# Two weight loads moved ahead of a wait and a row load on SyncE's queue

## The reference

```python
# 1. attention, q k v (2, 8, 768, 64): bits of q @ proj and k @ proj give a bucket; only equal buckets attend
scores = scale * q @ k.T;  scores = where(q_bucket == k_bucket, scores, -1e9)
x = (softmax(scores) @ v).transpose(0, 2, 1, 3).reshape(1536, 512)
# 2. SwiGLU with RMS norm, d_ff = 1536
xn = x / sqrt(mean(x * x) + 1e-6) * rms_g
x = (silu(xn @ w_gate) * (xn @ w_val)) @ w_out
# 3. one expert of eight for each token, w1[e] (512, 1024), w2[e] (1024, 512)
e_idx = argmax(x @ gate);  gate_w = the chosen probability;  eom = sigmoid(x @ output_gate)
out[e_idx == e] = gate_w * eom[:, e] * (relu(x[e_idx == e] @ w1[e]) @ w2[e])
```

## Time and profile before

| | |
|---|---|
| median of 3 runs | 762.18 us (761.68 to 762.22) |
| profiled execution, its time | 762.22 us |
| its span | 760.5 us |
| TensorE matmul busy | 744.0 us, 98% |
| chain that ended last, TensorE's share | 85% |

### The profile page before, as it was taken

The page is one execution under the profiler, slowest core; times in us unless marked ns, Lnnn a source line. Parts: engine busy times, 40 slices in busy tenths (PEclk is TensorE's granted clock), DMA queues, the critical chain, the costliest instruction groups (busy, mean ns, idle before and its releaser), DMA issues.

```text
span 760.5 us, 13422 instructions
## 1 busy us (share of the span) xinstructions
PE 744.0 (98%) x4556; PEld 678.6 (89%) x4556; DVE 475.6 (63%) x930; ACT 377.0 (50%) x675; POOL 300.9 (40%) x346
## 2 busy tenths in 40 slices
PE   6999999999999999999999999999999999999996
PEld 5899899989888999999999998888899988889985
DVE  8899999999987764344434453336366654665430
ACT  5988898888898411111111123443435454455531
POOL 7778777778888654433333200111110111010111
PEclk9999999999999999999999999999999999999998
DMA  7797788688410131121111022003046767776400
GB/s 216 208 277 210 212 238 211 191 196 223 118 34 29 35 118 42 56 66 45 41 41 41 0 97 83 29 28 139 33 160 207 227 199 239 258 219 200 157 25 23
DMA packets 54677, 98.33 MB, mean 129 GB/s; under 512 B 7042, under 2 KB 21390, under 8 KB 54625
## 3 DMA queue, kind: packets, MB, share of 16 engines
q1 hardware_dynamic: 50390, 87.69, 39.1%
q0 software_dynamic: 2240, 6.31, 2.4%
q10 hardware_dynamic: 1995, 3.65, 2.1%
HBM read 57.99 MB, written 22.89 MB: 106 GB/s over the span
## 4 chain that ended last, share of the span: by engine, by line
PE 85%; DVE 10%; issue 2%; ACT 2%; POOL 0%; POOLq 0%; DVEq 0%; ACTq 0%
PE ps_s L991 13%; PE ps_t L1149 13%; PE ps_s L1229 8%; PE ps_t L991 7%; PE ps_t L944 6%; PE ps_p L1244 6%; PE ps_t L1244 6%; PE ps_s L1234 4%; DVE pT_l L1597 4%; PE ps_o L991 3%; PE ps_p L991 3%; PE ps_s L929 3%; PE ps_s L930 3%; DVE negmax L1577 3%; PE ps_o L959 1%
## 5 line engine op out<-in xcount | busy, mean ns | idle before, releaser
L741 POOL TENSOR_SCALAR probs<-probs,rden,alone 128x768 f32<-128x768 f32 x95 | 92.8, 991 | 33.5 <-DVE rden L1591 33.5
L1597 DVE TENSOR_TENSOR pT_l<-ps_t,pT_h 128x384 fp32r<-128x384 f32 x192 | 97.5, 548 | 5.2 <-ACT pT_h L1304 4.1
L991 PE MATMUL ps_s<-xn,w_h 128*128 128x384 f32 x384 | 97.4, 334 | 0.0
L1294 ACT ACTIVATE probs<-ps_s,negmax 128x768 f32<-128x768 f32 x96 | 87.1, 907 | 16.9 <-DVE negmax L1577 15.9
L1577 DVE TENSOR_REDUCE negmax<-ps_s 128x1 f32<-128x770 f32 x96 | 90.8, 946 | 4.4 <-PE ps_s L930 3.6
L1304 ACT ACTIVATE pT_h<-ps_t 128x384 fp32r<-128x384 f32 x192 | 85.2, 491 | 15.6 <-PE ps_t L944 14.2
L944 PE MATMUL ps_t<-ident,probs 128*128 128x128 f32 x576 | 87.2, 282 | 3.2 <-DVE pT_l L1597 2.6
L944 PEld LDWEIGHTS ps_t<-ident,probs 128*128 128x128 f32 x576 | 63.2, 141 | 22.6 <-DVE pT_l L1597 10.4
L1772 DVE TENSOR_TENSOR expert_w<-piece,expert_w 128x2048 fp32r<-128x2048 f32 x32 | 72.5, 2288 | 17.3 <-ACT expert_w L1459 17.2
L870 POOL DMA_INDIRECT out_dram<-rows_out,rows_in x16 | 16.0, 1001 | 168.1 <-ACT rows_out L1489 168.1
L991 PEld LDWEIGHTS ps_s<-xn,w_h 128*128 128x128 f32 x384 | 69.3, 188 | 0.0
(11 more groups left out here) (286 smaller groups left out, 1684.8 us busy)
## 6 DMA issues: line engine op xcount, KB each, us to landing
piece<-in_moe_w_dram SPq DMA_DIRECT2D x32, 1024.0 KB, 5.6
routed<-filler SPq DMA_DIRECT2D x60, 257.0 KB, 4.7
k_a<-qk_h SPq DMA_DIRECT2D x28, 192.0 KB
rows_in<-routed ACTq DMA_DIRECT2D x7, 481.9 KB, 4.6
rawv<-in_v_dram SPq DMA_DIRECT2D x8, 384.0 KB, 6.0
w_raw<-in_moe_w_gate_dram SPq DMA_DIRECT2D x12, 256.0 KB, 3.1
w_raw<-in_moe_w_val_dram SPq DMA_DIRECT2D x12, 256.0 KB, 3.4
wo_raw<-in_moe_w_out_dram SPq DMA_DIRECT2D x12, 256.0 KB, 2.6
```

What stands on the lines that cost most here:

```text
L741: nc.gpsimd.tensor_scalar(pr, pr, rden[:, j:j + 1], alone[:, j:j + 1], ALU.mult, ALU.add).then_inc(norm_done, 4 - own if j % 3 == 1 else 1)
L991: mm = nc.tensor.matmul(unit_banks[tg][w][:, 0:G], a_[par][:, w, c, :], xn_at(tg, part, c), start=(n == 0), stop=(n == 3 * C - 1))
L1294: nc.scalar.activation(probs[:, j].rearrange("p (a n) -> p a n", a=2), third(ps_s[j % 2]), ACT.Exp, bias=negmax[:, j:j + 1], accum_out=psu ...
L1597: nc.vector.tensor_tensor(pT_l[u % 4][:], ps_t[kt % 2][:, 0:G], pT_h[u % 4][:].bitcast(F32), ALU.subtract).then_inc(low_ready, 1)
```

## The change

SyncE issues the loads of pieces (1, 2) and (1, 3) before it waits for the ten scatters and loads the early rows. Its own wait for the early rows is gone. Every other wait, also those inside `load_piece`, stays, and no other engine's code changes.

```diff
             sp.wait_ge(hs_low, NT)
             load_piece(0, 3)
+            load_piece(1, 2)
+            load_piece(1, 3)
             sp.wait_ge(scattered, 16 * (NT - LATE))
             sp.dma_start(rows_in[0][0:HALF, :, 0:DM], blocks_v[:, first_block(0), :, 0:DM]).then_inc(early_rows_in, 16)
-            sp.wait_ge(early_rows_in, 16)
-            load_piece(1, 2)
-            load_piece(1, 3)
             sp.wait_ge(late_scattered, 16 * LATE)
             sp.dma_start(rows_in[0][0:HALF, :, DM:DM + 2], blocks_v[:, first_block(0), :, DM:DM + 2],
                          allow_slow_non_contiguous=True).then_inc(rows_loaded[0], 16)
```

## The result

The changed kernel took 767.36 us in the median of 4 runs (766.53 to 767.87), the kernel before 762.20 us (761.68 to 762.53). The ratio is 1.0069, with a 95% interval of 1.0057 to 1.0083: 5.2 us slower, 4.3 to 6.3. The forecast was 762.3 us and no change. Over all 25 executions of the changed kernel on record, those beside the experiments included, the times go from 765.68 to 769.43 us.

A forecast was written before the change was run, and what follows sets the result against it. TensorE, 98% busy and 85% of the chain, was taken as the bound. Removed wait 0, later early rows +0.1 and GpSimd 0, added to 762.22, gave 762.3 us, with a range of 761.6 to 764.0.

The forecast's parts named there:

- GpSimd's third waiter: GpSimd's scatter of tile 10, also waiting for the early rows, would go at about 567.3 to 567.9; cost 0.
- The reading of the chain: From 564 to 596 us the chain was taken as TensorE nearly throughout, following on itself from 567.72 through the expert stage.
- no price up to about 567.1: At TensorE's line 1133: early rows landing by 567.1 cost nothing, each microsecond beyond costs a full one.
- The early rows behind piece (1, 3): On SyncE's queue, rows follow the piece and land at 566.6 to 567.7, taken as 567.2; price 0.1 us.
- the landing of (1, 3): Piece issued on SyncE's queue at 560.6 lands after 4.8 to 5.9 us, at 565.4 to 566.5.
- the burst's step: Three pieces issued almost together on SyncE's queue landed so that each further megabyte was taken to add 2.6 us.
- the rows' own share: The early rows' 480 KB behind piece (1, 3) were taken to add 1.2 us, scaled from 2.6 us per megabyte.
- The scatter: The tenth scatter, beside piece (1, 2), lands after 4.5 us instead of 3.0, so the early rows are issued at 562.3.
- Rival 1: Early rows take their whole 4.0 us behind piece (1, 3), landing at 569.6; price 2.5 to 3.4 us; chance 0.10.
- Rival 2: TensorE, waiting longer near 567, drops to half clock for 3.4 us, about 1.7 us on top; chance 0.03.
- Rival 3: Rows share the engines with piece (1, 3) rather than follow it, landing at 566.3 to 567.1; 762.2 us; chance 0.17.
- Rival 4: Moving 2 MB away from 565 to 574 us speeds something up there, a true gain over 1.5 us; chance 0.03.

The follow-up runs named there:

- the two on other numbers: Changed kernel with the early rows read from weights w2, and the same without SyncE's wait for the scatters; against the kernel before, ratios 1.0078 and 1.0071.
- TensorE kept at work: Changed kernel plus 24 extra transposes on TensorE before the early rows' first matmuls; 764.90 us, ratio 1.0039 against the kernel before.

## Why the prediction was wrong

**What held.** The removed wait was worth nothing: alone it gave +0.1 us. The pieces' own waits set their issues at 556.4 and 560.6; they went at 556.5 and 560.8. GpSimd's third waiter cost nothing: its scatters went at 571.91 and 576.91, and nobody on the chain waited for them. The chain passes a delay on whole: what was late at the early rows' matmuls was late at the end, with the clock's share added on the way, and behind 579 everything moved by the same 6.8 us. The reading of the chain had skipped a stretch, though. Between 567.72 and 572.23 it is not TensorE alone; VectorE holds it from 568.35 to 569.31 (choosing the expert for the last tile) and ScalarE from 571.52 to 572.10. Since they only follow on TensorE's work, this changed nothing. The landing had no price up to about 567.1: with (1, 2) alone the rows landed at 567.0 and TensorE did not wait.

**The step that failed** is "The early rows behind piece (1, 3)", with its landing of 566.6 to 567.7, where the profile shows 571.1. It put together two terms, and both were too small.

The larger is the landing of (1, 3), taken as 4.8 to 5.9 us from rows of pieces that were issued on idle engines. At 560.6 the engines were not idle: (1, 2) and, after it, the scatter of tile 9 were still to be moved. Measured, the piece needed 8.2 us in the two kernels that show it. Waiting in line does not explain this. (1, 2) landed at 562.0 and the scatter at 563.2, and the burst's step of 2.6 us for a piece behind a piece would then give a landing of (1, 3) at 564.6 to 565.8, inside or ahead of the forecast's 565.4 to 566.5. What the rows show in its place is that a piece issued while others were under way was moved unevenly: with the same rows behind it, it took 9.1 to 10.3 us from its issue to their landing in the changed kernel and the two on other numbers, and 7.3 to 7.4 us when it was issued on idle engines. Issuing it 2 us later, behind the scatters, cost nothing. The burst shows a piece issued 0.4 us behind another (7.1 us to landing); no row that I used shows one issued 4.2 us behind another, with a scatter between them.

The smaller is the rows' own share, 1.2 us by their bytes. Behind one piece on idle engines they landed 7.3 to 7.4 us after its issue, so 1.4 to 2.6 us after a piece that lands in 4.8 to 5.9. That they come in 2 KB packets, which I gave as the reason for a small addition, does not set them apart: the pieces do too (424 packets, 0.87 MB). But with the engines' share near 1 in both, 348 GB/s were moved while the piece flowed and 221 once the rows were under way (the stretches at 566 and 567 above); at 221 GB/s the rows' 0.49 MB take 2.2 us, not 1.2. With (1, 3) alone moved this was the only error, and 7.4 us from the piece's issue is 0.3 past the late end that I had given (5.9 + 1.2).

The scatter was mis-sized too, 5.3 us where 4.5 was taken, but the later issue of the rows did not matter: the kernel that issues them 1.7 us sooner lands at the same moment.

**The rivals.** Rival 1, with a chance of 0.10, gave a landing of 569.6 to 570.5 and 2.5 to 3.4 us; the wait alone measured +3.0. That it came near was luck, for its mechanism is not there: rows that pay their whole 4.0 us behind a piece would land 9.0 us after a piece issued on idle engines, and they landed after 7.3 to 7.4. They wait for a piece that is itself slow. Rival 2, the clock, had 0.03 and a price of 1.7 us on top. Once the wait is 2.6 us or more it was there in every profile, lasted 6.8 us and not 3.4, and measured 2.2 to 2.5 us. The two are not alternatives but a sum, 3.0 + 2.2 = 5.2, and I had priced them together only for a landing at 568. Rival 3, no order in the queue, was tested with a queue of the rows' own and is dead in this form: the engines were shared, and the rows were as late. Rival 4, faster, did not show either: no kernel gained. The Trainium skill, page "DMA: Bandwidth & Descriptors", section "Queues, rings and completion order", says that each DMA engine takes packets from its queue rows in turn. From 567 to 568 the trace of that kernel agrees, with 55.6% and 35.6% for the two queues. In the changed kernel it is not to be seen at the scatter of tile 9, whose instruction ended at 558.85. The queues from 558.6 to 560.9 (packets, MB, share of the engines):

```profile
DMA packets 424, 0.87 MB, mean 378 GB/s; under 512 B 0, under 2 KB 0, under 8 KB 424
...
q1 hardware_dynamic: 424, 0.87, 101.1%
```

All 424 packets are the piece's, on SyncE's queue; GpSimd's show up from 561 on.

**What stays open.** The tail. In the changed kernel's profile the DMA share is 0.26, 0.08 and 0.04 in the last three microseconds; that is 0.38 us of sixteen engines, which an even load would have done by about 568.4. A few engines were far behind the others, by up to 3 us in that execution and less in others. Neither the rows' table, their queue nor their issue makes it. The five profiles that have it (the changed kernel, the rows on ScalarE's queue, TensorE kept at work, and the two on other numbers) are those in which (1, 3) was issued while (1, 2) and the scatter were under way. In the profile with both pieces issued together from 560 and in the one with (1, 3) behind the scatters, the share went from 0.85 and 0.94 in one microsecond to 0.07 and 0.14 in the next. So the tail goes with that overlap; which engine falls behind, and why, no run here shows.

## What to carry to other kernels

Before a load is moved ahead of a small one that somebody needs soon, add up what will be on the DMA engines at that moment, from all queues, and take every landing time from a row with the same load in front of it: the landing time of a DMA on idle engines (4.8 to 5.9 us here) says little about one that is issued while others are under way (8.2). A load that nobody waits for belongs behind the one that is waited for, even if its buffer is free earlier. And a new wait of TensorE has two prices, the wait and the clock behind it; work out whether the clock falls for each size of the wait, not for the likeliest alone.

## What the runs showed of the hardware

- The granted clock fell in each of the six profiles with a wait of TensorE of 2.6 to 4.0 us, and stayed down for about 6.8 us (from about 571.0 to 577.9 in the changed kernel), against 3.4 us in the first microseconds of the kernel before. It did not fall with waits of 0.45 to 0.89 us in the profiles taken.
- A 1 MB load and the 480 KB load behind it landed 7.3 to 7.4 us after the first one's issue on idle DMA engines, and 9.1 to 10.3 us after it where another 1 MB load and a scatter were under way. In the second case the DMA share was 0.35 or less in the last two microseconds before the landing.
- 24 useless transposes of 128x128, 2.78 us of TensorE's time in a wait, made the kernel 2.5 us faster than the changed one.
- A scatter of 257 KB on GpSimd's queue, issued 1.4 us behind a 1 MB load on SyncE's, landed after 4.9 to 5.8 us instead of 2.7 to 3.1, in all profiles with that pair.
- A second DMA's issue on SyncE took 0.5 to 1.0 us, against 0.37, where a 1 MB load had been issued right ahead of it.
